# Pooled query, key and value sums made by accumulating DMAs, and the split of the weights given to GpSimd, in an attention plus two-layer MLP kernel

## The chip, the cores and the metric

The kernel runs on one core of one Trainium2 chip. The metric is the device time of one execution in microseconds (us). The core's engines are named as the profile names them: PE (TensorE, matrix multiplies), DVE (VectorE), ACT (ScalarE), POOL (GpSimd) and SP (SyncE, which here only issues DMAs). Each engine runs its own list of instructions in order and waits for semaphores that others count up.

## The reference

Four batches, eight heads, 576 positions, head dimension 64. Attention is the sum of two parts: a pooled one on averages of four consecutive positions, and a local one in a band. Two MLP layers follow.

```python
q_d = q.reshape(B, H, Sd, factor, D).mean(axis=3)       # k_d, v_d alike; factor 4, Sd 144
out_up = np.repeat(sm_attn(q_d, k_d, v_d), factor, axis=2)
mask = np.abs(pos[:, None] - pos[None, :]) < factor
scores = np.where(mask, scale * np.matmul(q, k.transpose(0, 1, 3, 2)), -1e9)
out_local = np.matmul(softmax(scores), v)
x = (out_up + out_local)                                  # as 2304 tokens x 512
h = x @ w_in;   x = (h - np.tanh(h)) @ w_out              # 512 -> 2048 -> 512
h = x @ w2_in;  out = (h * np.cos(h)) @ w2_out
```

## The kernel before, in words

Every engine's program is written out by hand.

**Attention units.** The attention is cut into 36 units (`UNITS`): for each batch five local ones, of 116 queries over all heads, and four pooled ones, of 72 pooled queries over four heads. Batch 0 has units 0 to 8: local 0 to 3, pooled 4 to 7, local 8. Batch 1 has local 9 to 11, pooled 12 to 15, local 16 and 17. A unit goes through `scores` on PE, `top_score` and `maximum` on DVE, `exponentials` on ACT, `guard`, `invert` and `normalise` on DVE, `transposes` on PE, `evacuate` on ACT, `mixes` on PE and `gather` on DVE, which adds the result to x. In its `scores` a pooled unit reads `qd` and `kd`, in its `mixes` it reads `vd`: the sums of four rows of q, k and v (the average's factor is put into later scales).

**First stage.** Units 0 to 7 run before the MLP, in a loop over k on every engine. On PE, iteration k issues a few dummy matmuls on the tile `warm` (`keep_warm`, their number is in `FILL`, else 1), then `scores(k + 1)`, `mixes(k - 2)` and `transposes(k - 1)`. An instruction that waits holds up all behind it on its engine.

**The MLP.** The tokens are cut into six tiles of 384, the hidden dimension into 16 chunks of 128, so each layer has 96 steps s. PE's `hidden(s + 2)` computes h of a chunk, ACT takes tanh, DVE subtracts, ACT and DVE split g into a high and a low float32r part, and `contract(s)` multiplies by w_out. All products are made from three matmuls of such parts, so PE needs each weight as `hi` (rounded) and `lo` (the rest). The first layer's steps carry the remaining units between them: a unit's `scores`, its `transposes` and its `mixes` stand at places 0, 3 and 4 after its start, with two places a step and a new unit every five places.

**Weights.** They come in quarters of 1 MB: `w_in` quarter n serves `hidden` of chunks 4n to 4n+3, `w_out` quarter n serves `contract` of the same chunks, for the first time in tile 0. Each quarter is four pieces of 128x512. In the first layer the `hi` pieces are made by DVE (quarter 0 of w_in, `hi_piece`), by POOL (quarter 1 of w_in, `split_w`) and by ACT (all six others, `hi_pieces`, put between steps by `HI_ACT`); the `lo` pieces by POOL but for six that DVE makes. POOL makes all of the second layer's.

**Sums of four.** For batch 0 the rows are loaded whole (`load_fours`) and added by DVE (k, `pool_k`) and POOL (q, v, `sum_of_four`). For batches 1 to 3 they come in 16 chunks through two small buffers (`load_chunk`), SP loading a chunk when the one two before it is summed, POOL adding each with two instructions (`chunk`). For batch 1 POOL's chunks stand between its `lo` pieces, in one fixed order.

Of the kernel before, what the change touches and what calls it, by code (L numbers as in the profile page):

```python
# [95 lines left out]
CHUNKS = 16  # L96


def after(count):
    return count + CREDIT  # L100


def build(nc, qx, kx, vx, qf, kf, v4, w_in, w_out, w2_in, w2_out, const, out):
    with ExitStack() as ctx:
        sem = lambda name: ctx.enter_context(nc.semaphore(name))
        KB = 1024
        slab = ctx.enter_context(nc.sbuf_tensor("slab", [P, 821 * 64], F32))
# [50 lines left out]
        qf_ld, kf_ld = ([sem(f"{name}{hs}") for hs in range(2)] for name in ("qf_ld", "kf_ld"))  # L158
        v4_ld = [sem(f"v4_ld{c}") for c in range(2)]
        qk_ld = [sem(f"qk_ld{i}") for i in range(5)]  # L160
        v_ld = [sem(f"v_ld{i}") for i in range(5)]
        chunk_ld = [sem(f"chunk_ld{i}") for i in range(2)]
# [10 lines left out]
        pool_part, pooled, k_part, pooled_k = sem("pool_part"), sem("pooled"), sem("k_part"), sem("pooled_k")  # L173

        hi_dve, hi_act, hi_gp = sem("hi_dve"), sem("hi_act"), sem("hi_gp")
# [54 lines left out]
        HI_ACT = {-2: (0, True), 1: (1, True), 3: (2, False), 5: (2, True), 7: (3, False), 9: (3, True)}  # L230

        def hi_count(n, out_weights):
            return KC * list(HI_ACT.values()).index((n, out_weights))


# [12 lines left out]
        def _(sp):  # L248
# [15 lines left out]
            def load_chunk(b, n):  # L264
                g = (b - 1) * CHUNKS + n

                sp.wait_ge(pooled, after(12 + g - 1))
                if n < 8:
                    src = (qf, kf)[n // 4]
                    sp.dma_start(chunk_sb[g % 2][:, :], src[b, :, n % 4, :]).then_inc(chunk_ld[g % 2], 16)  # L270
                else:
                    c, cc = (n - 8) // 4, n % 4
                    sp.dma_start(chunk_sb[g % 2][0:QH, 0:512], v4[b, c, :, cc, :]).then_inc(chunk_ld[g % 2], 16)
# [24 lines left out]
            def load_fours(src, dst, ld, hs):  # L298
                pairs = slice(2 * hs, 2 * hs + 2)
                sp.dma_start(dst[:, pairs, :], src[0, :, pairs, :]).then_inc(ld[hs], 16)  # L300
# [20 lines left out]
            load_wi(0, 1, w_in)  # L321
            load_wo(0, 1, w_out)
            load_chunk(1, 0)
            load_chunk(1, 1)

            sp.wait_ge(pooled, after(12))
            load_wi(0, 2, w_in)
            sp.wait_ge(pooled_k, after(PAIRS))
            load_wo(0, 2, w_out)
            load_qk(9)  # L330
# [4 lines left out]
            load_v(9)  # L335


            chunk_at = {9: (1, 2, 2, 4), 10: (1, 4, 6, 8), 11: (1, 8, 10, 12), 12: (1, 12, 14, 16), 15: (2, 0, 2, 2),
                        17: (2, 2, 4, 6), 18: (2, 6, 8, 10), 19: (2, 10, 12, 14), 20: (2, 14, 16, 16), 25: (3, 0, 2, 2),
                        26: (3, 2, 4, 6), 27: (3, 6, 8, 10), 28: (3, 10, 12, 14), 29: (3, 14, 16, 16)}  # L340
            next_store = 0
            for u in range(FIRST + 1, NU):
                if 5 * (u - FIRST - 1) >= 2 * FC * (next_store + 1):
                    store_y(next_store)
                    next_store += 1
                more = u in LBUF and later_local(u) is not None
                if more:
                    load_qk(later_local(u))
                cb, c0, c1, c2 = chunk_at.get(u, (0, 0, 0, 0))
                for c in range(c0, c1):  # L350
                    load_chunk(cb, c)
                if more:
                    load_v(later_local(u))
                for c in range(c1, c2):
                    load_chunk(cb, c)
# [31 lines left out]
        def _(pe):  # L387
# [8 lines left out]
            def scores(u):  # L396
# [22 lines left out]
                else:  # L419
                    if b == 0:  # L420
                        pe.wait_ge(pooled, after(2 * hs + 2))
                        pe.wait_ge(pooled_k, after(2 * hs + 2))
                    else:
                        pe.wait_ge(pooled, after(12 + CHUNKS * (b - 1) + 8))
# [21 lines left out]
            def mixes(u):  # L446
# [14 lines left out]
                else:  # L461
                    pe.wait_ge(pooled, after(12 + CHUNKS * b if b else 8 + 4 * hs))
# [7 lines left out]
            def hidden(s):  # L470
# [11 lines left out]
                for kc in range(KC):  # L482
                    if c == 0:
                        pe.wait_ge(xl_done, after(KC * t + kc + 1))
                    if s == 0 and kc < 2:
                        pe.wait_ge(lo_dve, after(kc + 1))
# [8 lines left out]
            def contract(s):  # L495
                m, t, c = s // STEPS, s // FC, s % FC
                first, last = c == 0, c == FC - 1
                if t % TILES == 0 and c % 4 == 0:
                    if m == 0 and c >= 8:
                        pe.wait_ge(lo_dve, after(2 + c - 4))  # L500
                    else:
                        pe.wait_ge(wo_split, after((8 if m else 0) + c + 4))
# [40 lines left out]
            FILL = {0: 7, 1: 2, 2: 8, 3: 3}  # L543
# [40 lines left out]
        def _(sc):  # L584
# [70 lines left out]
            def hi_pieces(n, out_weights):  # L655
                if out_weights:
# [420 lines left out]
```

## Time and profile before

| | |
|---|---|
| time, median of 3 runs | 942.13 us (941.74 to 944.63) |
| the profiled execution's own time | 945.7 us |
| its span, first to last instruction | 943.8 us |
| PE busy | 916.4 us (97%) |
| DVE, ACT, POOL busy | 551.1, 389.5, 179.9 us |
| mean granted TensorE clock | 0.982 |

The span is the time between the first and the last instruction in the trace; the execution's own time has 1.9 us more around it. The granted clock is the share of full speed (2.4 GHz) at which TensorE was let run; 0.5 is the lower level, 1.2 GHz.

### The profile page before, as it was taken

What the parts mean: (1) busy time and instruction counts of PE and PEld (TensorE: products, weight loads), DVE (VectorE), ACT (ScalarE), POOL (GpSimd) and SP (SyncE); (2) the same over time, 40 slices, a digit from 0 to 9 for tenths busy, and PEclk for the clock granted to TensorE, in tenths of its full rate; (3) what the DMA queues carried; (4) which work ended last, traced back from release to release, by engine and by line L of the source; (5) the groups of instructions that cost most, each with busy time, mean ns of one, the idle gap of its engine ahead of it and who ended that gap; (6) DMA issues with size and microseconds to landing.
All of it is one profiled execution on the core that took longest, in us unless ns stands there. A gap on an engine that the chain in (4) does not pass through costs nothing.

```text
span 943.8 us, 15983 instructions
## 1 busy us (share of the span) xinstructions
PE 916.4 (97%) x6263; PEld 849.6 (90%) x6263; DVE 551.1 (58%) x1096; ACT 389.5 (41%) x1063; POOL 179.9 (19%) x214
## 2 busy tenths in 40 slices
PE   7798799999999999999999999999999999999998
PEld 5588689999999999999999999999999999999997
DVE  5854445444445444443225598677677777777765
ACT  5364524444434443343223244344344344444343
POOL 2577511142001420000038960000000000000000
PEclk9698989999999999999999999999999999999999
DMA  9934100243201430020024331001001000000000
GB/s 302 369 115 135 49 26 34 82 143 93 70 2 59 133 105 1 9 94 1 34 94 141 113 112 34 6 29 34 34 1 34 34 1 1 34 1 1 34 1 33
DMA packets 30530, 62.00 MB, mean 66 GB/s; under 512 B 2856, under 2 KB 6056, under 8 KB 30312
## 3 DMA queue, kind: packets, MB, share of 16 engines
q1 hardware_dynamic: 30456, 60.99, 19.3%
q8 instruction: 49, 0.80, 0.4%
q14 instruction: 25, 0.20, 0.1%
HBM read 51.54 MB, written 9.44 MB: 65 GB/s over the span
## 4 chain that ended last, share of the span: by engine, by line
PE 92%; DVE 3%; ACT 2%; DMA 1%; POOL 1%; issue 1%; SPq 0%; ACTq 0%; DVEq 0%
PE ps L491 41%; PE ps L538 21%; PE ps L519 21%; PE ps L417 2%; PE ps L466 1%; PE ps L458 1%; PE ps L427 1%; PE ps L442 1%; ACT pr_all L598 1%; DMA kb<-kx_in 1%; PE ps L436 1%; DMA chunk<-v_in 1%; DVE stats L734 1%; PE ps L411 0%; DVE stats L747 0%
## 5 line engine op out<-in xcount | busy, mean ns | idle before, releaser
L491 PE MATMUL ps<-xh,wi_hi 128*128 128x384 f32 x768 | 261.9, 341 | 0.0
L491 PE MATMUL ps<-xh,wi_lo 128*128 128x384 f32 x768 | 258.0, 336 | 0.0
L491 PE MATMUL ps<-xl,wi_hi 128*128 128x384 f32 x768 | 257.4, 335 | 0.0
L491 PEld LDWEIGHTS ps<-xh,wi_hi 128*128 128x128 f32 x768 | 144.3, 188 | 7.0 <-issue 1.3
L491 PEld LDWEIGHTS ps<-xl,wi_hi 128*128 128x128 f32 x768 | 144.3, 188 | 4.1
L491 PEld LDWEIGHTS ps<-xh,wi_lo 128*128 128x128 f32 x768 | 144.1, 188 | 0.0
L638 ACT ACTIVATE gh<-rem 128x384 fp32r<-128x384 f32 x96 | 50.5, 526 | 212.6 <-PE ps L538 141.7
L519 PE MATMUL ps<-gh,wo_hi 128*128 128x384 f32 x384 | 134.3, 350 | 2.1 <-DVE wo_lo L821 1.5
L519 PE MATMUL ps<-gl,wo_hi 128*128 128x384 f32 x384 | 130.0, 339 | 0.0
L519 PE MATMUL ps<-gh,wo_lo 128*128 128x384 f32 x384 | 129.9, 338 | 0.0
L834 DVE TENSOR_TENSOR fn<-ps,fn 128x384 f32<-128x384 f32 x96 | 53.3, 556 | 126.4 <-ACT fn L626 126.2
L538 PE MATMUL ps<-wo_hi,gl 128*128 128x512 f32 x288 | 113.9, 396 | 0.0
L538 PE MATMUL ps<-wo_lo,gh 128*128 128x512 f32 x288 | 113.7, 395 | 0.0
L538 PE MATMUL ps<-wo_hi,gh 128*128 128x512 f32 x288 | 111.9, 389 | 0.0
L626 ACT ACTIVATE fn<-ps 128x384 f32<-128x384 f32 x96 | 47.5, 495 | 145.9 <-PE ps L491 145.8
L850 DVE TENSOR_SCALAR fn<-ps 128x384 f32<-128x384 f32 x96 | 53.4, 556 | 63.4 <-PE ps L491 63.4
L598 ACT ACTIVATE pr_all<-ps,stats 128x64 f32<-128x64 f32 (+1 forms) x176 | 55.7, 337 | 78.9 <-DVE stats L740 78.9
L842 DVE TENSOR_TENSOR gl<-fn,gh 128x384 fp32r<-128x384 f32 x96 | 61.1, 636 | 42.4 <-ACT gh L638 42.2
L519 PEld LDWEIGHTS ps<-gh,wo_hi 128*128 128x128 f32 x384 | 73.1, 190 | 5.9 <-DVE wo_lo L821 1.8
L638 ACT ACTIVATE gh<-fn 128x384 fp32r<-128x384 f32 x96 | 50.7, 528 | 59.4 <-DVE fn L834 58.9
L967 POOL TENSOR_TENSOR chunk<-chunk 128x288 f32<-128x288 f32 (+1 forms) x48 | 39.4, 821 | 183.0 <-PE ps L427 86.9
L519 PEld LDWEIGHTS ps<-gh,wo_lo 128*128 128x128 f32 x384 | 73.3, 191 | 0.0
(90 smaller groups left out, 1238.9 us busy)
## 6 DMA issues: line engine op xcount, KB each, us to landing
wi_raw<-w_in_in SPq DMA_DIRECT2D x32, 256.0 KB, 4.8
wo_raw<-w_out_in SPq DMA_DIRECT2D x8, 1024.0 KB, 7.3
qb<-qx_in SPq DMA_DIRECT2D x20, 256.0 KB, 2.9
kb<-kx_in SPq DMA_DIRECT2D x20, 256.0 KB, 3.8
vb<-vx_in SPq DMA_DIRECT2D x20, 256.0 KB, 2.8
y_between<-stage SPq DMA_DIRECT2D x6, 768.0 KB, 4.6
x<-y_between SPq DMA_DIRECT2D x6, 768.0 KB, 4.6
out<-stage SPq DMA_DIRECT2D x18, 256.0 KB, 2.1
```

Source lines behind the costliest of these rows:

```text
L417: mm = MM(ps[rows, bank + slot // 4, slot % 4 * KW:(slot % 4 + 1) * KW], qb[i][rows, cols], kb[i][rows, cols], start=False, stop=(slot % 4 ...
L427: mm = MM(ps[0:QH, bank + h4 % 2, (h4 // 2) * SD:(h4 // 2 + 1) * SD], qd[rows, pair, n * QH:(n + 1) * QH], kd[rows, pair, :], start=True, ...
L491: mm = MM(ps[:, h_bank(s), 0:NT], w, xx[:, kc, :], start=(n == 0), stop=(n == last))
L519: mm = MM(ps[:, j, 0:NT], w[:, c % 4, cols], gg[:, :], start=(first and n == 0), stop=(last and n == 2))
L538: mm = MM(ps[:, out_bank(t, j), :], gg[:, cols], w[:, c % 4, :], start=(first and n == 0), stop=(last and n == 2))
L598: e = nc.scalar.activation(p_u[0:n, c * w:(c + 1) * w], src, ACT.Exp, scale=scale, bias=negmax[0:n, u % 2, c:c + 1], accum_out=sums[0:n, u ...
L626: nc.scalar.activation(fn[s % 2][:, :], ps[:, h_bank(s), 0:NT], ACT.Tanh).then_inc(f_done, 1)
L638: nc.scalar.activation(gh[s % 3][:, :], g[:, :], ACT.Copy).then_inc(gh_done, 1)
L834: nc.vector.tensor_tensor(fn[s % 2][:, :], h, fn[s % 2][:, :], ALU.subtract).then_inc(g_done, 1)
L842: nc.vector.tensor_tensor(gl[s % 3][:, :], g[:, :], gh[s % 3][:, :].bitcast(F32), ALU.subtract).then_inc(gl_done, 1)
L850: nc.vector.tensor_scalar(fn[s % 2][:, :], ps[:, h_bank(s), 0:NT], 1.0 / TWO_PI, MAGIC, ALU.mult, ALU.add).then_inc(u_done, 1)
L967: TT(rows[:, 0:2 * w], rows[:, 0:2 * w], rows[:, 2 * w:4 * w], ALU.add).then_inc(pool_part, 1)
```

## The change

Batches' sums of four are no longer added by engines. SP loads the first of the four rows straight into `kd`, `qd` and `vd` (`load_first_of_four`), and POOL then issues three DMAs for each of the three tiles that add the second, third and fourth row from memory onto it (`add_of_four`, `accum_op=ALU.add`); each waits until the one before it on the same tile has landed. A pooled unit's `scores` wait for all three sums of q and of k of the batch (`q_summed`, `k_summed`), its `mixes` for those of v. The chunk buffers, `load_chunk`, `load_fours`, `pool_k` and `sum_of_four` go.

The `hi` pieces of quarter 0 of w_in move from DVE to ACT, in iterations 6 and 7 of the first stage. All other quarters of both layers are split by POOL alone, `hi` then `lo` of each piece; ACT's `hi_pieces` and DVE's `lo_of_out` go. POOL's new order: nine accumulates of batch 0, the rest of quarter 0 of w_in, w_out 0, w_in 1, three accumulates of batch 1, w_out 1, three more, w_in 2, three more, w_out 2, w_in 3, w_out 3, then batches 2 and 3. SP's loads of quarters 2 and 3 now stand behind `load_first_of_four(1)`, which waits for unit 7. `FILL` has one more dummy matmul ahead of the scores of each of units 5, 6 and 7.

```diff
-            def load_chunk(b, n):
...
+            def load_first_of_four(b):
+                if b:
+                    sp.wait_ge(scored, after(LAST_POOLED[b - 1] + 1))
+                sp.dma_start(kd[:, :, :].rearrange("p a s -> p (a s)"), kf[b, :, 0, :]).then_inc(k_first, 16)
+                sp.dma_start(qd[:, :, :].rearrange("p a s -> p (a s)"), qf[b, :, 0, :]).then_inc(q_first, 16)
+                if b:
+                    sp.wait_ge(mixed, after(LAST_POOLED[b - 1] + 1))
+                sp.dma_start(vd[0:QH, :, :].rearrange("p c n -> p (c n)"), v4[b, 0]).then_inc(v_first, 16)
...
             sp.dma_start(const_sb[:, :], const).then_inc(const_ld, 16)
             load_qk(0)
+            load_first_of_four(0)
             load_qk(1)
             load_v(0)
-            load_fours(kf, kf_0, kf_ld, 0)
-            load_fours(qf, qf_0, qf_ld, 0)
             load_qk(2)
...
-            load_fours(kf, kf_0, kf_ld, 1)
-            load_fours(qf, qf_0, qf_ld, 1)
             load_v(3)
-            for c in range(2):
-                sp.dma_start(v4_0[c][0:QH, :, :], v4[0, c]).then_inc(v4_ld[c], 16)
...
+                for b in range(1, B - 1):
+                    if u == LAST_POOLED[b] + 2:
+                        load_first_of_four(b + 1)
...
-                    if b == 0:
-                        pe.wait_ge(pooled, after(2 * hs + 2))
-                        pe.wait_ge(pooled_k, after(2 * hs + 2))
-                    else:
-                        pe.wait_ge(pooled, after(12 + CHUNKS * (b - 1) + 8))
+                    pe.wait_ge(q_summed, 48 * (b + 1))
+                    pe.wait_ge(k_summed, 48 * (b + 1))
...
-                    pe.wait_ge(pooled, after(12 + CHUNKS * b if b else 8 + 4 * hs))
+                    pe.wait_ge(v_summed, 48 * (b + 1))
...
-            FILL = {0: 7, 1: 2, 2: 8, 3: 3}
+            FILL = {0: 7, 1: 2, 2: 8, 3: 3, 5: 2, 6: 2, 7: 2}
...
-                if s in HI_ACT:
-                    hi_pieces(*HI_ACT[s])
...
+                if k in (6, 7):
+                    hi_piece(2 * k - 12)
+                    hi_piece(2 * k - 11)
...
-                if k in (1, 3):
-                    pool_k(k - 1)
-                    pool_k(k)
...
-                if s in (6, 7):
-                    lo_of_out(2, 2 * s - 12)
...
+            def add_of_four(b, f):
+                n = 16 * (3 * b + f - 1)
+                if f == 1:
+                    gp.wait_ge(k_first, 16 * (b + 1))
+                else:
+                    gp.wait_ge(k_summed, n)
+                gp.dma_start(kd[:, :, :].rearrange("p a s -> p (a s)"), kf[b, :, f, :], accum_op=ALU.add).then_inc(k_summed, 16)
...
+            for f in range(1, FACTOR):
+                add_of_four(0, f)
```

ACT's list in the first layer, from the evacuation of unit 9 on, in the program before (`gh` is `g_hi`, `fn` is tanh, `pr_all<-ps` of 128x512 is `evacuate`, `pr_all,stats<-ps,stats` is `exponentials`):

```order
L608 ACTIVATE pr_all<-ps 128x512
L638 ACTIVATE gh_71<-fn_78 128x384
L667 ACTIVATE wo_hi_61<-wo_raw_53 128x512 x4
L626 ACTIVATE fn_77<-ps 128x384
L598 ACTIVATE pr_all,stats<-ps,stats 128x64 x8
L638 ACTIVATE gh_72<-fn_77 128x384
L626 ACTIVATE fn_78<-ps 128x384
L638 ACTIVATE gh_73<-fn_78 128x384
L667 ACTIVATE wi_hi<-wi_raw 128x512 x4
L608 ACTIVATE pr_all<-ps 128x512
L626 ACTIVATE fn_77<-ps 128x384
```

The same stretch of ACT's list in the changed program:

```order
L573 ACTIVATE pr_all<-ps 128x512
L603 ACTIVATE gh_71<-fn_78 128x384
L591 ACTIVATE fn_77<-ps 128x384
L563 ACTIVATE pr_all,stats<-ps,stats 128x64 x8
L603 ACTIVATE gh_72<-fn_77 128x384
L591 ACTIVATE fn_78<-ps 128x384
L603 ACTIVATE gh_73<-fn_78 128x384
L573 ACTIVATE pr_all<-ps 128x512
L591 ACTIVATE fn_77<-ps 128x384
```

The two blocks of four `hi` pieces are gone; the second of them stood directly ahead of unit 10's evacuation.

POOL's list ahead of the first weights, in the changed program (before, 12 pairs of `TENSOR_TENSOR` on q and v stood here, 24 instructions):

```order
L899 DMA kd<-kf_in 128x576
L904 DMA qd<-qf_in 128x576
L909 DMA vd<-v_in 72x1024
L899 DMA kd<-kf_in 128x576
L904 DMA qd<-qf_in 128x576
L909 DMA vd<-v_in 72x1024
L899 DMA kd<-kf_in 128x576
L904 DMA qd<-qf_in 128x576
L909 DMA vd<-v_in 72x1024
L929 ISA
L929 TENSOR_TENSOR wi_lo<-wi_raw,wi_hi 128x512 x2
```

Nine transfers now stand where engine work on batch 0's q and v stood, each three of one tile one after the other.

## Rows read from the trace of the kernel before

**Rows 1.** Windows: us, busy (instructions) of engines, PEclk, DMA share, GB/s

```profile
8.00:16.00 8.00, 7.20 (x95) 5.80 (x95) 4.99 (x12) 5.86 (x37) 2.98 (x4) 1.00 1.03 403
16.00:24.00 8.00, 6.19 (x154) 4.51 (x150) 7.45 (x21) 6.96 (x40) 3.16 (x5) 1.00 1.04 252
...
80.00:90.00 10.00, 7.62 (x81) 7.22 (x82) 2.63 (x7) 3.23 (x7) 6.67 (x8) 0.66 0.26 85
90.00:126.00 36.00, 27.82 (x195) 25.48 (x193) 13.17 (x27) 16.03 (x48) 18.64 (x23) 0.86 0.23 72
126.00:540.00 414.00, 413.87 (x3235) 398.05 (x3234) 183.39 (x362) 158.33 (x508) 90.71 (x111) 1.00 0.21 69
540.00:944.00 404.00, 400.44 (x2009) 362.52 (x2007) 300.82 (x600) 170.26 (x322) 18.98 (x18) 1.00 0.07 25
```

**Rows 2.** Timeline of PE: start, us, line, [idle before, releaser]

```profile
66.49 0.69 PE L458 MATMUL ps<-pr_all,vb 64*64 64x58 f32 x32
...
82.38 1.12 PE L458 MATMUL ps<-pr_all,vb 64*64 64x58 f32 x32 [2.39 <-ACT pr_all L608]
...
107.88 0.44 PE L519 MATMUL ps<-gh,wo_hi 128*128 128x384 f32 x1 [1.47 <-DVE wo_lo L821]
...
119.57 1.25 PE L466 MATMUL ps<-pr_all,vd 72*64 72x72 f32 x16 [6.71 <-POOL vd L970]
...
135.28 0.77 PE L466 MATMUL ps<-pr_all,vd 72*64 72x72 f32 x16
```

**Rows 3.** Chain that ended last, 66 to 130 us: start, us, what

```profile
67.18 2.28 PE ps L491 x12
...
83.50 4.14 PE ps L519 x12
...
91.79 2.08 PE ps L519 x12
...
120.82 4.14 PE ps L519 x12
124.97 1.17 PE ps L427 x8
```

**Rows 4.** Timeline of ACT around 80 us

```profile
79.67 2.17 ACT L667 ACTIVATE wi_hi<-wi_raw 128x512 fp32r<-128x512 f32 x4
81.75 0.57 ACT L608 ACTIVATE pr_all<-ps 128x512 f32<-128x512 f32 x1
```

**Rows 5.** The same chain, ahead of the wait at 119.57

```profile
105.96 3.01 POOL wi_lo L993
...
111.66 2.56 DMA chunk<-v_in
```

**Rows 6.** The chain in the first stage, 0 to 66 us

```profile
5.12 7.57 DMA kb<-kx_in
...
19.69 0.67 PE ps L427 x8
...
21.98 0.51 DVE kf L807
...
23.40 0.31 DVE kd L809
...
34.01 0.53 PE ps L394
...
38.78 0.67 DVE wi_hi L813 x2
```

**Rows 7.** DMA issues in 0 to 50 us: KB each, median us to landing

```profile
wi_raw<-w_in_in SPq DMA_DIRECT2D x16, 256.0 KB, 9.5
...
const_sb<-const_in SPq DMA_DIRECT2D x1, 160.0 KB, 2.3
```

**Rows 8.** Timeline of POOL, one quarter of w_out in layer two

```profile
516.23 0.63 POOL L997 TENSOR_SCALAR wo_hi<-wo_raw 128x512 fp32r<-128x512 f32 x1
...
524.71 0.62 POOL L997 TENSOR_SCALAR wi_hi<-wi_raw 128x512 fp32r<-128x512 f32 x1
```

More of the change, by code:

```diff
@@ L484, in hidden @@
                         pe.wait_ge(xl_done, after(KC * t + kc + 1))
-                    if s == 0 and kc < 2:
-                        pe.wait_ge(lo_dve, after(kc + 1))
+                    if s == 0 and kc >= 2:
+                        pe.wait_ge(lo_dve, after(kc - 1))
+                    elif s == 0:
+                        pe.wait_ge(wi_split, after(kc + 1))
                     elif t % TILES == 0 and c % 4 == 0:
@@ L498, in contract @@
                 if t % TILES == 0 and c % 4 == 0:
[L499 to L502, printed above, removed]
+                    pe.wait_ge(wo_split, after(16 * m + c + 4))
                 pe.wait_ge(gh_done, after(s + 1))
@@ L653, in evacuate_out, with hi_piece @@
                         nc.scalar.activation(stage2[:, j, :], ps[:, out_bank(t, j), :], ACT.Copy).then_inc(ev_act, 1)
[L655 to L667 removed]
+            def hi_piece(c):
+                sc.wait_ge(wi_ld[0][0], 16 * KC)
+                nc.scalar.activation(wi_hi_of(0, c), wi_raw[:, c, :], ACT.Copy).then_inc(hi_act, 1)
             for k in range(FIRST + 2):
@@ L959, in _ @@
         def _(gp):
-            for s in (pool_part, pooled, hi_gp, wi_split, wo_split):
+            for s in (hi_gp, wi_split, wo_split):
                 gp.sem_inc(s, CREDIT)
             TT = nc.gpsimd.tensor_tensor
-            counts = {"part": 0, "pooled": 0, "hi": 0}
-            def sum_of_four(rows, w, dst):
-                TT(rows[:, 0:2 * w], rows[:, 0:2 * w], rows[:, 2 * w:4 * w], ALU.add).then_inc(pool_part, 1)
-                counts["part"] += 1
-                gp.wait_ge(pool_part, after(counts["part"]))
-                TT(dst, rows[:, 0:w], rows[:, w:2 * w], ALU.add).then_inc(pooled, 1)
-                counts["pooled"] += 1
@@ L1014, in _ @@
-            for pair in range(PAIRS):
-                gp.wait_ge(qf_ld[pair // 2], 16)
-                sum_of_four(qf_0[:, pair, :], SD, qd[:, pair, :])
-            for hs in range(2):
-                for c in range(2):
-                    gp.wait_ge(v4_ld[c], 16)
-                    for cc in (2 * hs, 2 * hs + 1):
-                        sum_of_four(v4_0[c][0:QH, cc, :], P, vd[0:QH, c, cc * P:(cc + 1) * P])
-            for c in range(2, KC):
-                gp.wait_ge(hi_dve, after(c + 1))
-                lo_piece(0, c, False)
@@ new lines, in split_wi, with split_wo @@
+            def split_wi(m, n):
+                gp.wait_ge(wi_ld[m][n], 16 * KC)
+                for i in range(n * KC, (n + 1) * KC):
+                    nc.gpsimd.tensor_scalar(wi_hi[:, i, :], wi_raw[:, i, :], 1.0, 1.0, ALU.mult, ALU.mult).then_inc(hi_gp, 1)
+                    gp.wait_ge(hi_gp, after(next(pieces)))
+                    TT(wi_lo[:, i, :], wi_raw[:, i, :], wi_hi[:, i, :].bitcast(F32), ALU.subtract).then_inc(wi_split, 1)
+            def split_wo(m, n):
+                gp.wait_ge(wo_ld[m][n], 16)
+                for c in range(KC):
+                    nc.gpsimd.tensor_scalar(wo_hi[n][:, c, :], wo_raw[n][:, c, :], 1.0, 1.0, ALU.mult, ALU.mult).then_inc(hi_gp, 1)
+                    gp.wait_ge(hi_gp, after(next(pieces)))
+                    TT(wo_lo[n][:, c, :], wo_raw[n][:, c, :], wo_hi[n][:, c, :].bitcast(F32), ALU.subtract).then_inc(wo_split, 1)
@@ new lines, in _ @@
+            for f in range(1, FACTOR):
+                add_of_four(0, f)
+            for c in range(2):
+                gp.wait_ge(hi_act, after(c + 1))
+                TT(wi_lo[:, c, :], wi_raw[:, c, :], wi_hi_of(0, c).bitcast(F32), ALU.subtract).then_inc(wi_split, 1)
+            split_wo(0, 0)
+            split_wi(0, 1)
+            add_of_four(1, 1)
+            split_wo(0, 1)
+            add_of_four(1, 2)
+            split_wi(0, 2)
+            add_of_four(1, 3)
+            gp.wait_ge(mixed, after(FIRST))
@@ L1036, in _ @@
+            split_wo(0, 2)
+            split_wi(0, 3)
+            split_wo(0, 3)
             for b in (2, 3):
-                for n in range(CHUNKS):
-                    chunk(b, n)
+                for f in range(1, FACTOR):
+                    add_of_four(b, f)
             for n in range(WG):
-                split_w(1, n, False)
-                split_w(1, n, True)
+                split_wi(1, n)
+                split_wo(1, n)
 def kernel(q, k, v, moe_w_in, moe_w_out, moe2_w_in, moe2_w_out):
```

140 lines of the change are left out of this document (23 added, 117 removed).

## The prediction

> **What bounds the kernel now.** I read the windows first [rows 1]: from 126 us on PE is busy in all but 0.1 us of 414 and in all but 3.6 of 404, at full clock. Nothing there waits for weights or sums, and the changed kernel gives PE the same matmuls in the same order. So the change is worth what it does to the moment at which that solid block begins: what PE gains or loses before 126 us comes out at the end one for one. Second, PE's timeline before 126 us [rows 2]. In the MLP's first steps it shows three gaps: 2.39 us before the mixes of unit 10 (released by ACT's evacuation), 1.47 before a `contract` (DVE's `lo` pieces) and 6.71 before the mixes of unit 12 (POOL's last v sum of batch 1). Third, the chain [rows 3]: right after the first and the third gap a `contract` takes 4.14 us where it takes 2.08 elsewhere, and the windows of these two places show granted clocks of 0.66 and 0.86 where their neighbours show 1.00 [rows 1]: after idling, PE ran at 1.2 GHz for some 6 us. After the 1.47 us gap no such stretch follows. Last, the chain of the first stage [rows 6], which runs through loads, DVE and PE alternately; there DVE is busy 7.45 of 8 us [rows 1].
>
> **Taken away in the MLP's first steps.** (a) The gap at 82.38: ACT did four `hi` pieces in 2.17 us directly ahead of the evacuation that PE waited for [rows 4]. They go, so 2.2 us of the 2.39 go. (b) The gap at 107.88 waited for DVE's `lo` pieces of w_out, which go: 1.5 us. (c) The gap at 119.57: the chain ahead of it is POOL's `lo` piece, itself waiting for ACT's `hi`, then v chunks with a DMA of 2.56 us between them [rows 5]. In the new order batch 1's nine accumulates are issued ahead of w_out 2, and should be complete some 20 us before that unit's mixes (below): 6.7 us. (d) The half clock behind (a) and (c): twice a `contract` at 4.14 for 2.08, so 4.1 us; mixes at 1.12 for 0.69 and 1.25 for 0.77 [rows 2], 0.9; scores at 1.17 for 0.67 [rows 3, 6], 0.5; together 5.5. Sum: 2.2 + 1.5 + 6.7 + 5.5 = 15.9 us.
>
> **Does POOL bring the weights in time?** A quarter split by POOL alone takes 8.5 us (516.23 to 524.71, eight instructions) [rows 8]. POOL begins once ACT's first `hi` pieces are done in iteration 6; unit 8's dummy matmul, in iteration 7 on PE, is at 34.01 by the old times [rows 6], so I take 35. Two `lo` pieces take 2.6, w_out 0 is ready at 46, w_in 1 at 55; three accumulates to issue, taken at 1 us each, w_out 1 at 67; three more, w_in 2 at 78; three more, then w_out 2 at 90, w_in 3 at 98, w_out 3 at 107. PE first wants w_in 1 at 67.2 and w_out 1 at 83.5 [rows 3]; w_in 3 it wants two quarters after w_in 1, right after the scores at 124.97 [rows 3], which is 59 us, or 43 without the gaps and the half clock of above. So each quarter comes 21.5 us after the last one, and the slack is 12 us or more at each, and a first stage that ends later moves both sides, because POOL's start hangs on ACT's place in the same stage. So I cost POOL's extra `hi` work (16 pieces in layer one) at nothing; what hides it is that slack. If each issue held POOL some 2 us longer than the 1 us taken, w_out 2, behind nine of them, would be late first. Batch 3's first row can be loaded eleven places ahead of the scores that need it: five and a half steps of two blocks of 2.08 us, 23 us at least, for a load and three accumulates. I cost that at nothing too.
>
> **Added in the first stage.** Unit 4's scores were at 19.69 [rows 6]. Now they wait until three accumulates of k and of q have landed one after the other, and the mixes of unit 1 and the transposes of unit 2 are queued behind them on PE; DVE and ACT wait for those. The first row of k follows constants and unit 0's loads in SP's queue, about 1 MB in all; with the constants landing 2.3 us after their issue [rows 7] and, say, some 300 GB/s after that (between the 252 and 403 of rows 1), q's first row lands near 7.4 us. Three accumulates of L us then end at 7.4 + 3L. No row shows an accumulating DMA or any DMA of POOL. Bounds from rows: L is at least 2.3 (a small transfer on an idle chip) and at most 9.5 (a w_in piece behind SP's backlog [rows 7]). The DMA engines are full in this time, 403 GB/s at best [rows 1], and a round of the three tiles moves 0.88 MB: 2.2 us with all of the bandwidth, 4.4 with half of it. A wait queue of its own should spare them SP's backlog but not the sharing, so I take 5.5, nearer to the sharing than to the backlog. Sums ready at 23.9: 4.3 us later than 19.6. Below L = 4 nothing is lost, as the other loads hold unit 4 until then.
>
> The Trainium skill ("DMA: Bandwidth & Descriptors", Queues, rings and completion order) says that a DMA engine takes turns between the queues it has work for, packet by packet. By that rule POOL's transfers get half of the engines whatever SP has queued; as an estimate from that page it would put L nearer 4.4 and the loss near 1 us.
>
> **Taken away in the first stage.** DVE's second pair of `pool_k` lay on the chain from 21.98 to 23.71: 1.7 us. Two `hi` pieces of w_in on DVE lay on it at 38.78: 0.7 [rows 6]. Their twins on ACT stand where it waits for PE anyway. The three dummy matmuls cost up to 0.53 each at the low clock [rows 6], 1.4 in all; if they keep the clock up they cost less. Net of the stage: +4.3 - 1.7 - 0.7 + 1.4 = +3.3 us.
>
> **Sum.** -15.9 + 3.3 = -12.6 us on a span of 943.8: 931.2, an execution of its own of 933.1. The median of the runs is 3.6 below the profiled execution's 945.7, so the timed median should be 942.13 - 12.6 = 929.5 us.
>
> **Rivals.** (1) The sums don't gate: L of 4 or less. Then the stage gains 1 us instead of losing 3.3, -16.9 in all, and up to 4 more if PE, no longer idle there, gets full clock in the stage: 921 to 925. For it: the first rows stand early in SP's queue. Against: engines that are full by 8 us.
>
> (2) The sums come as slowly as SP's backlog: L of 8 to 9.5 gives sums at 31 to 36 us, a stage that ends 11 to 15 us later than before, and 937 to 942. Slower than before it gets from L = 9.9 on, which is just past my upper row, but an add reads its target as well as its source, and no row bounds that. At L = 11 it gives 945.5. This is the case on the other side; its place is unit 4's scores.
>
> (3) Engine work on the same memory blocks POOL while it writes a transfer's descriptors. DVE is busy 7.45 of 8 us in this stage, in instructions such as the two `hi` pieces in 0.67 and an add in 0.51 [rows 6]; one such block for each of the nine issues is up to 6 us on POOL, of which three to six reach the chain: sums at 27 to 30 us, 932 to 936. The Trainium skill ("SBUF — State Buffer", the "DVE blocks DMA" trap) speaks against the change in just this way: a GpSimd-issued DMA stands while VectorE holds the port that both use, and its example grows from 0.62 to 3.1 us. As an estimate from that page, 2.5 us more for each of three rounds puts the median near 937.
>
> (4) POOL becomes the bound: an accumulate keeps POOL for its whole 5.5 us instead of 1. Then w_in 2 is ready at about 105 instead of 78, w_out 2 at 130, where PE wants it near 105, and 20 us or more of waiting eat the gain: 940 to 955. From about 4 us an issue on the wait outweighs the 12.6 us gained. Against: a DMA's issue on SP's queue takes far less than its landing.
>
> **Chances.** My forecast (L of 4 to 7, POOL in time) 0.48; rival 1 0.18; rival 3 0.13; rival 2 0.12, of which a quarter is at or past no change; rival 4 0.06, half of it slower; 0.03 for other mishaps. About 0.3% (2.8 us) is what a measurement of this kernel can tell from no change. Faster 0.87, same 0.05, slower 0.08. The likeliest case alone spans 925 to 934; with rivals 1 and 3 and the better part of 2 the range is 921 to 939.
>
> **What the changed trace would show.** Right: no gap above 1 us on PE between its first `hidden` and the old 126 us mark, no 4.14 us `contract`, and the first `hidden` starting near 51 instead of 48 us, with a gap before unit 4's scores released by an accumulate into `qd` near 24 us. Wrong: that gap absent or twice as long (L), a gap at a `hidden` or `contract` released by POOL's `lo` pieces (rival 4), or gaps of the attention's small steps that the old stalls covered. The forecast fails most easily on L: each microsecond of it is three in the end.

## The result

| | before | after |
|---|---|---|
| time, median of 6 runs each, same chip | 942.95 us (941.74 to 944.63) | 938.53 us (936.78 to 939.05) |
| ratio to before, 95% interval | | 0.995 [0.9935, 0.9965] |
| the profiled execution: own time, span | 945.7, 943.8 us | 939.05, 937.3 us |
| mean granted clock | 0.982 | 0.987 |

The change gains 4.4 us in the medians and 6.5 in the spans of the two profiled executions; 12.6 were forecast. The profiled execution of the kernel before lay 2.8 us above the median of its runs and that of the changed kernel 0.5, so some 2 of the 6.5 us belong to these two executions and not to the change; no row says in which stretch. The windows of the changed kernel:

```profile
8.00:16.00 8.00, 5.71 (x54) 4.55 (x49) 2.69 (x7) 3.63 (x24) 2.61 (x3) 0.79 1.07 292
16.00:24.00 8.00, 5.95 (x114) 4.50 (x112) 4.22 (x11) 5.90 (x36) 2.60 (x3) 1.00 1.08 285
24.00:32.00 8.00, 0.04 (x2) 0.07 (x2) 0.00 (x0) 1.35 (x10) 1.72 (x2) 0.55 1.10 289
...
48.00:58.00 10.00, 6.38 (x55) 5.04 (x53) 9.84 (x14) 3.97 (x14) 9.67 (x9) 0.71 0.14 37
58.00:70.00 12.00, 10.03 (x106) 8.55 (x105) 8.97 (x14) 4.03 (x16) 11.63 (x12) 0.96 1.01 347
70.00:80.00 10.00, 10.00 (x88) 9.42 (x87) 5.06 (x8) 4.78 (x21) 9.71 (x11) 1.00 0.68 161
80.00:90.00 10.00, 10.00 (x86) 9.76 (x85) 5.37 (x9) 4.88 (x21) 9.67 (x11) 1.00 0.67 149
90.00:120.00 30.00, 30.00 (x278) 27.87 (x277) 15.13 (x29) 10.92 (x38) 26.71 (x26) 1.00 0.30 66
120.00:540.00 420.00, 419.97 (x3270) 404.22 (x3270) 181.52 (x367) 161.60 (x514) 69.05 (x70) 1.00 0.25 69
```

Two things are to be seen against [rows 1]. From 70 us on PE is never idle (to 0.03 us in 420) and its clock is full, where before there were three gaps and two stretches at the lower clock: that part came out as forecast. And from 24 to 32 us PE and DVE do nothing while the DMA engines are full: that is the new wait. It stands in PE's timeline of the changed kernel, with the two marks that I use from here on, the first `hidden` (57.97) and unit 9's scores (66.91):

```profile
31.96 1.24 PE L393 MATMUL ps<-kd,qd 64*72 64x144 f32 x8 [8.60 <-DMA qd<-qf_in]
...
52.12 1.18 PE L408 MATMUL ps<-eye_r,pr 72*72 72x72 f32 x8 [2.15 <-DVE pr L715]
...
57.97 0.52 PE L459 MATMUL ps<-xh,wi_hi 128*128 128x384 f32 x1
...
60.05 0.44 PE L459 MATMUL ps<-xh,wi_hi 128*128 128x384 f32 x1 [0.42 <-DVE xl L766]
...
63.19 0.66 PE L402 MATMUL ps<-eye_r,pr_all 128*128 128x128 f32 x4 [1.47 <-DVE pr_all L715]
...
66.91 1.15 PE L386 MATMUL ps<-kb,qb 64*64 64x64 f32 x32
```

The same two marks in the kernel before:

```profile
48.12 0.33 PE L491 MATMUL ps<-xh,wi_hi 128*128 128x384 f32 x1
...
54.81 1.15 PE L417 MATMUL ps<-kb,qb 64*64 64x64 f32 x32
```

The gap of 1.47 us at 63.19 lies behind the first `hidden`; the prediction said that there would be none above 1 us. DVE ended it and the one of 2.15 (below, e4). Before the change unit 4's scores were at 19.69 [rows 6]. The chain of the changed kernel shows what PE waited for, q's first row and then three accumulates one after the other:

```profile
2.60 5.57 DMA qd<-qf_in
...
8.46 8.47 DMA qd<-qf_in
...
17.22 7.48 DMA qd<-qf_in
...
24.98 6.89 DMA qd<-qf_in
...
31.96 1.24 PE ps L393 x8
```

The account of the 6.5 us by these marks:

| stretch | before | after | difference | forecast |
|---|---|---|---|---|
| start to unit 4's scores | 19.69 | 31.96 | +12.3 | +4.3 |
| from there to unit 9's scores | 35.12 | 34.95 | -0.2 | -1.0 |
| from there to the end of the span | 889.0 | 870.4 | -18.6 | -15.9 |

### The profile page after: what moved, and what is told of

Read it like the earlier page. It is cut to its first block, busy times and chain, and to the rows that moved or that the text cites. A ratio compares the mean times of both kernels' runs of the same rounds, so it can differ in the third digit from the quotient of the medians.

```text
span 937.3 us, 15833 instructions
## 1 busy us (share of the span) xinstructions
PE 912.2 (97%) x6266; PEld 845.4 (90%) x6266; DVE 540.8 (58%) x1076; ACT 379.6 (40%) x1043; POOL 161.3 (17%) x162
## 2 busy tenths in 40 slices
DMA packets 30409, 61.99 MB, mean 66 GB/s; under 512 B 2944, under 2 KB 6144, under 8 KB 30336
## 3 DMA queue, kind: packets, MB, share of 16 engines
q1 hardware_dynamic: 25728, 50.37, 16.1%
q0 software_dynamic: 4608, 10.62, 6.4%
## 4 chain that ended last, share of the span: by engine, by line
PE 94%; DMA 3%; DVE 2%; issue 0%; SPq 0%; ACT 0%
PE ps L459 43%; PE ps L484 22%; PE ps L503 21%; DMA qd<-qf_in 3%; PE ps L386 2%; PE ps L424 1%; PE ps L393 1%; PE ps L432 1%; PE ps L402 1%; PE ps L408 1%; DVE xl L766 1%; PE ps L380 0%; DVE pr L715 0%; PE ps L363 0%; DVE stats L690 0%
## 5 line engine op out<-in xcount | busy, mean ns | idle before, releaser
L781 DVE TENSOR_TENSOR gl<-fn,gh 128x384 fp32r<-128x384 f32 x96 | 58.8, 612 | 42.4 <-ACT gh L603 42.1
L484 PEld LDWEIGHTS ps<-gl,wo_hi 128*128 128x128 f32 x384 | 72.1, 188 | 0.0
```

What stands on the lines that cost most here:

```text
L484: mm = MM(ps[:, j, 0:NT], w[:, c % 4, cols], gg[:, :], start=(first and n == 0), stop=(last and n == 2))
L781: nc.vector.tensor_tensor(gl[s % 3][:, :], g[:, :], gh[s % 3][:, :].bitcast(F32), ALU.subtract).then_inc(gl_done, 1)
```

## The experiments

All of them are the changed kernel with one edit, unless a text says otherwise. This table gathers their marks, each from one profiled execution, in us; "tail" is the span less unit 9's scores. Each ratio is taken against runs of the kernel before that were made beside that kernel's own; their medians went from 942.95 to 944.36, so medians of different rows compare to about 1 us.

| kernel | median | ratio to before | unit 4's scores | first `hidden` | unit 9's scores | span | tail |
|---|---|---|---|---|---|---|---|
| before | 942.95 | 1 | 19.69 | 48.12 | 54.81 | 943.8 | 889.0 |
| after | 938.53 | 0.995 | 31.96 | 57.97 | 66.91 | 937.3 | 870.4 |
| e1: batch 0 by engines | 928.69 | 0.9837 | 19.38 | 49.91 | 58.49 | 928.8 | 870.3 |
| e2: weights held back | 935.12 | 0.9906 | 28.62 | 54.43 | 63.39 | 933.7 | 870.3 |
| e3: no adding | 935.58 (one run) | | 28.97 | 54.08 | 63.03 | 933.8 | 870.8 |
| e4: POOL later | 935.36 | 0.9909 | 31.98 | 55.52 | 62.56 | 933.8 | 871.2 |
| e5: v last | 947.76 | 1.003 | 32.03 | 61.93 | 71.00 | 941.6 | 870.6 |
| e6: no new dummies | 937.98 | 0.9941 | 32.18 | 56.67 | 65.78 | 936.2 | 870.4 |
| e7: e1 and e4 | 926.54 | 0.9821 | 19.75 | 45.81 | 52.86 | 924.1 | 871.2 |
| e8: e2 and e3 | 929.31 (one run) | | 25.06 | 49.45 | 57.28 | 927.5 | 870.2 |
| e9: ACT's `hi` back | 939.22 | 0.9949 | 31.37 | 54.91 | 61.99 | 937.0 | 875.0 |
| e10: e7 without dummies | 927.66 | 0.9824 | 19.44 | 47.02 | 54.07 | 925.4 | 871.3 |

Of the eleven kernels in which POOL issues the sums' transfers, all but e9 have a tail of 870.2 to 871.3. Within 1 us, whatever is lost ahead of unit 9's scores is lost one for one, and the MLP's gain is one number that can be read by itself.

### e1: batch 0's sums made by the engines

```diff
+            load_fours(kf0, kf_0, kf_ld, 0)
+            load_fours(qf0, qf_0, qf_ld, 0)
...
+                    if b == 0:
+                        pe.wait_ge(pooled, after(2 * hs + 2))
+                        pe.wait_ge(pooled_k, after(2 * hs + 2))
...
-            for f in range(1, FACTOR):
-                add_of_four(0, f)
+            for pair in range(PAIRS):
+                gp.wait_ge(qf_ld[pair // 2], 16)
+                sum_of_four(qf_0[:, pair, :], SD, qd[:, pair, :])
```

> Batch 0's sums are made by DVE and GpSimd as in the kernel before; batches 1 to 3 by accumulates, weights split by GpSimd as in the changed kernel. Theory (the changed kernel loses 12 us to three accumulates of 7 to 8.5 us in a row ahead of unit 4's scores, and gains 18 us in the MLP's first steps): unit 4's scores near 19.7 us instead of 32.0, first hidden near 48 instead of 58, time near 928 us. Rival (the wait is only replaced, by weights or by DVE slowed by GpSimd): first hidden after 54, time above 933.

Measured: 928.69 us (927.97 to 930.77), ratio 0.9837 [0.9815, 0.986]. Unit 4's scores are back at 19.38, the tail is unchanged, and the loss of the change is found: nearly 10 us of it are batch 0's accumulates. But the first `hidden` comes at 49.91, later than before (48.12), and unit 9's scores 3.7 us later (58.49 against 54.81), so something else costs time there. Two things show in its trace: DVE's `wi_lo` pair ahead of it takes 2.53 us where it took 1.28 before (e4 is on this), and the granted clock is 0.61, 0.50 and 0.50 in the three windows from 24 to 48 us, where the kernel before has 0.71, 0.65 and 0.57. This execution, at 930.77 us, is the slowest of the five.

### e2 and e3: what makes an accumulate long

e2 keeps SP's weights out of the way of batch 0's sums; e3 lets POOL's transfers (k and v alike) overwrite instead of add, so that the pooled part is made from every fourth row alone.

```diff
+            sp.wait_ge(q_summed, 48)
             load_wi(0, 0, w_in)
```

> The changed kernel, but SP issues the first weights only when batch 0's q sums have landed, so that no backlog shares the DMA engines with them beyond the first units' loads. Theory sharing (each accumulate of 7.6 us is long because SP's queue holds the engines): an accumulate of q takes 4 to 5.5 us, sums complete at 21 to 25 us. Rival (an accumulate is slow by itself, as the 5.7 to 6.4 us medians of batches 2 and 3 say): at least 6 us each, sums complete at 27 us or later.

```diff
-                gp.dma_start(..., accum_op=ALU.add).then_inc(q_summed, 16)
+                gp.dma_start(...).then_inc(q_summed, 16)
```

> The changed kernel, but GpSimd's transfers overwrite their target instead of adding to it (so the pooled part is computed from the fourth rows alone). Theory sharing: a transfer still takes 7 us or more with SP's backlog there. Rival (the adding costs): 3 to 5 us each, unit 4's scores at 20 to 24 us; the q0 queue's share per MB falls from 0.60% to about the 0.32% of SP's queue.

Measured: e2 935.12 us (934.69 to 935.54), ratio 0.9906 [0.9883, 0.9928]; e3 935.58 in its one run. In PE's timelines of e2, and then of e3, the wait shrinks from 8.60 to 5.20 and 6.84:

```profile
28.62 1.24 PE L394 MATMUL ps<-kd,qd 64*72 64x144 f32 x8 [5.20 <-DMA qd<-qf_in]
```

```profile
28.97 1.24 PE L393 MATMUL ps<-kd,qd 64*72 64x144 f32 x8 [6.84 <-DMA qd<-qf_in]
```

Sharing with the weights costs 3.3 us over the three rounds, adding 3.0. Neither theory held as written: with the weights held the sums came at 28.6 and not by 25 (the rival said 27 or later, at least 6 us each; the third took 4.99), and without the adding at 28.9, between the 7 us or more a round of the one and the 20 to 24 us of the other. The DMA queues from 0 to 36 us (packets, MB, share of 16 engines' time) show what adding takes. First the changed kernel, then e3:

```profile
q1 hardware_dynamic: 3876, 7.27, 61.4%
q0 software_dynamic: 1152, 2.65, 38.6%
```

```profile
q1 hardware_dynamic: 4930, 9.23, 76.7%
q0 software_dynamic: 768, 2.65, 21.2%
```

The same 2.65 MB take 1.8 times the engine time, and 1152 packets instead of 768, when they are added, and SP's queue moves less meanwhile (7.27 MB against 9.23).

### e8: neither adding nor sharing

The edits of e2 and e3 together.

> GpSimd's transfers of batch 0 to 3 don't add but overwrite (so the pooled part of the attention is computed from every fourth row alone), and SP's weight loads are held back until q's third transfer has landed: neither the adding nor the sharing with SP's weights is left. Holding alone brought unit 4's scores from 32.0 to 28.6 us, not adding alone to 29.0. If adding and sharing are separate costs they add up, the three transfers take about 5 us each and the scores come near 25 us. If both act through the same thing (engine time per round), one of them is enough: the scores stay near 28 us and what is left is three serial round trips of GpSimd-issued transfers, about 6 us each, which no relief of the DMA engines shortens.

Measured: 929.31 us in its one run. Its chain:

```profile
2.60 5.71 DMA qd<-qf_in
...
8.61 5.78 DMA qd<-qf_in
...
14.67 6.57 DMA qd<-qf_in
...
21.53 3.44 DMA qd<-qf_in
...
25.06 1.24 PE ps L394 x8
```

The two costs add up (3.3 + 3.0 = 6.3; the two together 6.9), so each acts on its own. What is left is 5.6 us a round, issue included ((25.06 - 8.31) / 3), for plain transfers that share the engines only with the loads of the attention. Only the last, with nothing of SP's in the way but v, comes down to 3.44. No run took the attention's loads away as well, so how much of the 5.6 is theirs stays open.

### e5: v's accumulates after k's and q's

```diff
-            for f in range(1, FACTOR):
-                add_of_four(0, f)
+            for f in range(1, FACTOR):
+                add_of_four(0, f, "kq")
+            for f in range(1, FACTOR):
+                add_of_four(0, f, "v")
```

> The changed kernel, but of batch 0 the three accumulates of k and q go first and v's three follow them, so that two tiles share a round (0.59 MB) where three did (0.88 MB). If a round is long because its transfers share the DMA engines, k's and q's accumulates take about 6 us each instead of 7.5, unit 4's scores come near 27 us instead of 32, and since v is wanted only some 10 us later, at most 3 us are given back there: a median 2 to 5 us below the changed kernel's 938.5, so 933.5 to 936.5. Rival: each accumulate has a fixed length of some 7 us whatever shares it (it took 6.6 to 7.0 with SP's weights held back). Then unit 4's scores stay at 30 to 32 us, v's sums land near 50 us instead of 32 and unit 4's mixes wait for them: 940 or more.

Measured: 947.76 us (941.56 to 950.57), ratio 1.003 [1.001, 1.0049]; its profiled execution is one of the shorter ones. My theory fell and the rival held. POOL's timeline shows it:

```profile
8.88 0.88 POOL L904 DMA_DIRECT2D qd<-qf_in  x1 [0.65 <-DMA qd<-qf_in]
...
17.31 0.86 POOL L904 DMA_DIRECT2D qd<-qf_in  x1 [1.31 <-DMA qd<-qf_in]
...
25.00 0.86 POOL L904 DMA_DIRECT2D qd<-qf_in  x1 [1.26 <-DMA qd<-qf_in]
25.53 1.21 POOL L904 DMA_DIRECT2D vd<-v_in  x1
34.60 0.84 POOL L904 DMA_DIRECT2D vd<-v_in  x1 [7.86 <-DMA vd<-v_in]
42.70 0.84 POOL L904 DMA_DIRECT2D vd<-v_in  x1 [7.26 <-DMA vd<-v_in]
```

q's issues stand 8.4 and 7.7 us apart with two tiles in a round, 8.8 and 7.8 with three in the changed kernel. v's own took 8.8, 7.8 and 4.6; the last two were alone in their rounds, the 7.8 while SP's weights still went on. The engines' time that v left went to SP's queue, not to k and q: from 0 to 36 us SP's queue moved 8.46 MB where it moved 7.27. And then PE waits at unit 4's mixes too, by its timeline:

```profile
47.44 1.25 PE L432 MATMUL ps<-pt,vd 72*64 72x72 f32 x16 [3.79 <-DMA vd<-v_in]
```

So while SP has weights to load, an accumulate of this size took 6.9 to 8.8 us whether one, two or three tiles shared its round. Putting them one behind the other costs; fewer at a time save nothing.

### e4: POOL begins its first quarter after DVE's split of x

```diff
+            gp.wait_ge(xl_done, after(KC))
             split_wo(0, 0)
             split_wi(0, 1)
```

> The changed kernel, but GpSimd begins with w_out's first quarter only when DVE has split x of tile 0. Theory (GpSimd's adds and splits slow DVE's instructions with both inputs in SBUF: the four splits of x took 4.7 us instead of 1.95): the splits take 2 us again, the step from the first hidden to unit 9's scores shrinks from 8.6 to 6.3 us, 1 to 3 us faster than the changed kernel, if the weights, now 10 us later, still have slack. Rival (no slack): a gap ahead of hidden(4) or contract(4) released by GpSimd, and no gain or a loss.

Measured: 935.36 us (934.74 to 936.27), ratio 0.9909 [0.989, 0.9927]. DVE's split of x ahead of the first `hidden`, in the timelines of the changed kernel and of e4:

```profile
52.66 2.64 DVE L761 TENSOR_TENSOR wi_lo<-wi_raw,wi_hi 128x512 fp32r<-128x512 f32 x2
...
56.09 4.79 DVE L766 TENSOR_TENSOR xl<-x,xh 128x384 fp32r<-128x384 f32 x4
```

```profile
50.68 1.28 DVE L761 TENSOR_TENSOR wi_lo<-wi_raw,wi_hi 128x512 fp32r<-128x512 f32 x2
...
53.64 1.96 DVE L766 TENSOR_TENSOR xl<-x,xh 128x384 fp32r<-128x384 f32 x4
```

The same instructions take over twice as long when POOL splits weights beside them: 4.79 against 1.96, and 2.64 against 1.28. POOL pays as well; a `hi` piece of it takes up to 1.66 us there and 0.63 in [rows 8]. With POOL held, unit 9's scores come 4.4 us earlier, the gaps of 2.15 and 1.47 that DVE ended are gone (0.39 is left of the first), and no gap for weights appears, so POOL's slack was real. Some of it is given back: a gap of 0.83 that DVE ended comes at 71.00, with POOL splitting weights beside it, and the tail is 871.2. So the span gains 3.5 and the median 3.2. Before the change POOL stood idle at this point of the program, by its timeline:

```profile
53.39 5.32 POOL L993 TENSOR_TENSOR wo_lo<-wo_raw,wo_hi 128x512 fp32r<-128x512 f32 x4 [11.59 <-ACT wo_hi L667]
```

That wait of 11.59 us for ACT's `hi` pieces had kept POOL off DVE's back, and the change took it away. In e9, where POOL waits for ACT again (14.47 us, until 60.74), DVE's split of x is back to 1.95 us and unit 9's scores come at 61.99, though nothing there makes POOL wait for DVE.

Not every instruction of DVE suffers: `x<-x,ps` of 128x352, which reads one operand from PSUM, takes 0.52 us in both kernels, in the changed one at 55.35 with a `hi` piece of POOL beside it (54.72 to 55.77).

The Trainium skill ("SBUF — State Buffer", SBUF: two separate sides) says that VectorE, in an operation with two inputs from SBUF, and a GpSimd operation that reads SBUF lock a shared pair of ports for a whole instruction, and the other waits. The trace agrees: the subtractions, with both inputs in SBUF, are slowed and the add with one in PSUM is not. The rule stood there to be applied to POOL's weights; I weighed only its other half, the trap about issuing DMAs. That half doesn't show in batch 0's issues: the first took 1.05 us and the other eight 0.85 to 0.89, with DVE busy from 0.00 to 4.22 of 8 us.

Two SBUF inputs are not the whole of it. DVE's `maximum`, a `TENSOR_SCALAR` of 128x8 with one tensor as input, takes 0.17 us in the mean from 120 us on. In e9 one took 3.42 us, and ended at 82.31, where a block of four subtractions of POOL ended (82.25); DVE's timeline, then POOL's:

```profile
78.89 3.42 DVE L711 TENSOR_SCALAR stats<-stats 128x8 f32<-128x8 f32 x1
```

```profile
76.24 6.01 POOL L932 TENSOR_TENSOR wo_lo<-wo_raw,wo_hi 128x512 fp32r<-128x512 f32 x4
```

In e7 a `guard` of 72x4, likewise a `TENSOR_SCALAR`, took 2.33 us and ended at 38.90, POOL's pair of subtractions beside it at 38.87. So a tiny instruction of DVE can stand behind several of POOL's in a row.

### e6: without the three new dummy matmuls

```diff
-            FILL = {0: 7, 1: 2, 2: 8, 3: 3, 5: 2, 6: 2, 7: 2}
+            FILL = {0: 7, 1: 2, 2: 8, 3: 3}
```

> The changed kernel without the three dummy matmuls that it adds in iterations 5 to 7 of the first stage. The prediction put them at +1.4 us. By that, the first hidden comes 1.4 us earlier and the median is 937.1. Rival: they hold up the granted clock in the stage and cost nothing on balance; then the windows from 32 to 58 us show a lower clock without them and the time is the same or up to 2 us longer (938.5 to 940.5).

Measured: 937.98 us (937.57 to 939.01), ratio 0.9941 [0.9926, 0.9957]: in the time not to be told from the changed kernel; in the trace 1.1 us less span, and from unit 4's scores to unit 9's 33.6 us where it was 34.95. The size is near the forecast's +1.4, but it is one execution against one, and the medians are 0.55 apart.

### e7: both losses taken out

The edits of e1 and e4 together.

> Batch 0's sums are made by the engines as before the change, the accumulates stay for batches 1 to 3, and GpSimd starts its first quarter of weights only after DVE's split of x. If the two losses found so far are separate (10 us for the late sums of batch 0, 3.2 us for DVE slowed beside GpSimd), this is 928.7 - 2.5 to 3.2: 925.5 to 926.2, DVE's x split takes 1.96 us instead of 4.22, and no gap for weights appears before 126 us, since GpSimd's slack was 12 us or more. Rival: the two overlap, or GpSimd, which has batch 0's q and v sums to make as well, now brings w_in 1 or w_out 1 too late: 928.5 or more, with a gap at a hidden or a contract released by GpSimd.

Measured: 926.54 us (925.67 to 927.65), ratio 0.9821 [0.9802, 0.9841], the fastest kernel of this study. The second loss can be taken out on top of the first: each of the five times lies below all five of e1, and the median is 2.2 us below (1.5 by the ratios, whose intervals overlap), where 2.5 to 3.2 were expected. DVE's split is back to 1.96 us, and PE waits for no weights. Unit 9's scores come 5.6 us before those of e1's trace, but that trace is of e1's slowest execution.

### e10: e7 without the dummies

The edits of e7 and of e6 together.

> Batch 0's sums by the engines, GpSimd held until DVE has split x, and without the three added dummy matmuls. If the dummies cost what they did in the changed kernel (1.3 us of the first stage), the median is 926.5 - 1.3 = 925.2. Rival: here PE doesn't idle for 8 us ahead of them, so they hold the clock up (the granted clock was 1.00 from 8 to 40 us with them), and without them the stage gets a lower clock: 926.5 to 928.

Measured: 927.66 us (926.29 to 928.01), ratio 0.9824 [0.9806, 0.9842]. By the times alone it can't be told from e7, but here the trace goes the other way than in e6: unit 9's scores 1.2 us later without the dummies. The windows from 24 to 40 us, first of e7, then of e10 (the number after the five engines is the granted clock):

```profile
24.00:32.00 8.00, 5.83 (x98) 4.04 (x90) 7.51 (x16) 4.76 (x20) 6.48 (x10) 1.00 1.03 313
32.00:40.00 8.00, 4.26 (x81) 3.45 (x80) 7.07 (x13) 4.11 (x13) 6.64 (x9) 1.00 1.04 382
```

```profile
24.00:32.00 8.00, 5.98 (x66) 4.34 (x62) 6.97 (x13) 3.45 (x15) 6.74 (x11) 0.70 1.04 332
32.00:40.00 8.00, 6.93 (x86) 5.76 (x84) 7.58 (x11) 5.47 (x18) 5.65 (x8) 0.66 0.99 367
```

In this execution of e7, with the dummies, PE stays at 2.4 GHz through both windows; in that of e10, without them, it spends most of them at 1.2. But e1 has the same dummies and, up to 37 us, the same program as e7, and its windows are:

```profile
24.00:32.00 8.00, 5.50 (x55) 3.98 (x55) 6.53 (x15) 2.03 (x9) 7.53 (x13) 0.61 1.05 386
32.00:40.00 8.00, 7.72 (x73) 5.85 (x72) 5.07 (x8) 6.24 (x22) 7.05 (x8) 0.50 0.92 342
```

So the clock here differs from execution to execution, and the dummies don't secure it. That they help is hinted at by the mean granted clocks of all executions (0.987 to 0.996 in the ten of e1 and e7, 0.987 to 0.991 in the four of e10), and not shown. In the changed kernel the clock is below full from 32 to 40 us with them or without (0.60 and 0.75).

### e9: how much of the MLP's gain is the weights'

```diff
+                if s in HI_ACT:
+                    hi_pieces(*HI_ACT[s])
...
+                    gp.wait_ge(hi_act, after(KC + KC * act_order.index((n, out_weights)) + c + 1))
...
+                if m == 0 and n >= 2:
+                    return lo_of_act(n, False)
...
+                if m == 0:
+                    return lo_of_act(n, True)
```

> The changed kernel, but ACT makes the hi pieces of w_out 0 and 1, w_in 2, w_out 2, w_in 3 and w_out 3 at the places where it made them before the change, and GpSimd only subtracts. So of the MLP's gain what the accumulates bring stays, and what the other split of the weights brings goes. In seven kernels so far the time from unit 9's scores (first kb,qb matmul after the first hidden) to the end is 870.2 to 871.2 us, in the kernel before the change 889.0. By the prediction's terms ACT's hi pieces cost 2.2 us of gap and the half clock behind it, 2.7 us or so: that stretch is 875 us here. GpSimd also starts later, which frees DVE's split of x as in the kernel with GpSimd held (3.2 us), so the median is 938.5 + 4.9 - 3.2 = 940.2. Rival: the weights' split costs nothing in itself, the gap at 82.38 came from GpSimd's v sums and lo pieces holding things up elsewhere; then the stretch stays at 870 to 871 and the median is 935.3.

Measured: 939.22 us (938.32 to 939.7), ratio 0.9949 [0.9933, 0.9965], and a tail of 875.0, as expected. ACT's timeline, and PE's with the wait that comes of it:

```profile
87.39 2.17 ACT L631 ACTIVATE wi_hi<-wi_raw 128x512 fp32r<-128x512 f32 x4
89.47 0.57 ACT L573 ACTIVATE pr_all<-ps 128x512 f32<-128x512 f32 x1
```

```profile
90.09 0.69 PE L424 MATMUL ps<-pr_all,vb 64*64 64x58 f32 x32 [1.30 <-ACT pr_all L573]
```

It is the picture of [rows 4]: four `hi` pieces ahead of an evacuation, but this wait is 1.30 of the 4.6 us. The rest is gaps of 1.48 and 0.59 that DVE ended, 0.65 that POOL's `lo` pieces ended, and small ones. The 1.48, at 86.04, follows the `maximum` of 3.42 us shown under e4: ACT waited 5.01 us for it. So this part of the loss is again DVE beside POOL, whose blocks now stand at other places. No stretch at half clock follows, so the size agrees with the expectation but is made up in another way: more waiting, no slow clock.

## Why the prediction was wrong

**The step that failed** is "so I take 5.5", the length of an accumulate. It was 8.5, 7.5 and 6.9, 7.6 in the mean. The sums came at 31.9 where the prediction said 23.9, which alone cost 8.0 us: 6.3 by L (three times 2.1), 0.8 by the first row, which landed at 8.16 instead of 7.4, and 0.9 by the 0.3 us between a landing and the next issue, for which the prediction has no term. The other terms gave 1.9 back, and that leaves the 6.1 us by which the span missed the forecast. The form "7.4 + 3L" held but for this last; L was mis-sized. I took 5.5 as a cost of bytes and shared bandwidth alone. Counted with its issue a round took 7.9 us ((31.96 - 8.16) / 3). Of these, plain transfers beside the attention's loads need 5.6 (e8), the adding puts 1.0 on them (e3), the weights in SP's queue 1.1 (e2), and 0.2 goes only with both. The bound named for it, "no row bounds that" of an add that reads its target, was the place to put weight. The reasoning by bytes in a round (0.88 MB, 2.2 to 4.4 us) was wrong in kind as well: two thirds of the bytes took nearly the same time (e5: 16.1 us for two rounds, 16.5 in the changed kernel).

**Rival 2** is what happened, by size and place. It asked for L of 8 or more, sums from 31 us on, and gave 937 to 942; L was 7.6 (7.9 with the issue), the sums came at 31.9 and the time is 938.5. Of its reasons, SP's backlog and an add that reads its target, the runs give 1.1 and 1.0 us a round to each; most of the length is there without either (e8). It had a chance of 0.12. The range of 921 to 939 holds the time only at its end.

**Rival 1** (sums don't gate) and **rival 4** (POOL as the bound) are excluded by the gap of 8.60 us and by the absence of any later one.

**Rival 3** (DVE blocks the writing of descriptors) is excluded for batch 0: the issues took 0.85 to 1.05 us, and the third accumulate of q was 6.9 us long while DVE did nothing (0.00 of 8 us from 24 to 32).

The Trainium skill ("DMA: Bandwidth & Descriptors", Queues, rings and completion order) has the engines take turns between queues. That by itself, as the prediction estimated from it, would have given L near 4.4; with 38.6% of the engines' time from 0 to 36 us POOL's queue did get a large share, and still an accumulate took 7.6 us.

**Terms (a) to (d)** gave -15.9, and the tail shows -18.6. Their direction and place were right: no gap and no half clock after 70 us. Two small gaps that the prediction left out, 0.49 at 58.76 and 0.60 at 63.82, are gone too, and make 1.1 of the 2.7 us more; the rest isn't accounted for, and the profiled execution of the kernel before was a long one. Of the 18.6, 4.6 come back when ACT makes the `hi` pieces again (e9), though not by the wait and the half clock of (a) and (d) alone; the other 14.0 are the accumulates', with DVE's `lo` pieces of w_out, which I didn't separate.

**POOL in time, at no cost** held for PE: nothing waits for weights. (Its slack "12 us or more at each" was 10.7 for w_in 2 by the prediction's own numbers, 67.2 + 21.5 - 78; that changed nothing.) What I did not see is that POOL at work is itself a cost: the sentence that costs the extra `hi` work "at nothing; what hides it is that slack" looked at who waits for POOL, not at who works beside it. e4 puts this at 3.2 us in the median and 4.4 at unit 9's scores.

**The net of the first stage** after unit 4 was forecast at -1.0 and is -0.2, in which the 4.4 us of DVE's slowing are contained; without them it would be about -4.6, so some 3.6 us were gained there that the prediction has no term for. The granted clock differs as well: 0.71, 0.65 and 0.57 in the 24 us from 24 to 48 before, 0.60, 1.00 and 0.71 in the 26 us from 32 to 58 after; what that is worth was not measured. The dummies' +1.4 (three times up to 0.53 is 1.6) agrees with the one trace of e6. Which part of the rest is DVE's and POOL's freedom from batch 0's sums was not measured on its own.

## What to carry to other kernels

Hand sums to accumulating DMAs where a serial chain of them has room: in batches 1 to 3 they cost nothing and took work off the path; at the start, with three in a row on the path and the queues full, each one took 7.6 us and engine sums were 10 us better (e1). When work moves to an idle engine, ask who shares memory with it at that moment, and let it start only when the neighbour's urgent work is done (e4, e7). And look for a mark after which all variants run alike: here the tail of 870 to 871 us made every experiment readable to 1 us.

## What the runs showed of the hardware

- An accumulating DMA of 288 KB, SBUF += memory, is slower also where SP's queue holds only the attention's loads and no weights. DMA issues from 180 to 235 us (KB each, median us to landing), of the changed kernel and of e3:

```profile
kd<-kf_in POOLq DMA_DIRECT2D x3, 288.0 KB, 5.6
qd<-qf_in POOLq DMA_DIRECT2D x3, 288.0 KB, 5.7
```

```profile
kd<-kf_in POOLq DMA_DIRECT2D x3, 288.0 KB, 4.1
qd<-qf_in POOLq DMA_DIRECT2D x3, 288.0 KB, 4.2
```

- Queue by queue over the whole of the changed kernel: 10.62 MB added took 6.4% of the engines' time, 50.37 MB of plain transfers 16.1%, so a megabyte added costs 1.9 times a plain one. Issuing one took POOL 0.85 to 0.92 us where it waited ahead of it (the very first 1.05), a plain one 0.54 to 0.63 (the first 0.74). Batch 1's stand one behind the other: 0.92, 1.20 and 1.56, overlapping, the three in 2.7 us.
- Removing a third of POOL's bytes from a round changed its length by 0.3 us at most (e5): what sets it while SP's queue is full is not the round's own bytes.
- DVE's subtraction of two SBUF tiles runs 2.4 times slower beside POOL's weight split (4.79 against 1.96 us for four). A `TENSOR_SCALAR` of 128x8 took 3.42 us instead of 0.17, until POOL's block of four subtractions was over (e9).
- The granted clock of a stretch is not fixed by the program: from 24 to 32 us, where e1 and e7 run the same program, the one execution was granted 0.61 and the other 1.00. What three dummy matmuls are worth there can't be read from one execution of each kernel.
